# The second product of each layer by seven products instead of eight, in ten of twelve runs

## What is computed

```
scores = q_c @ k_c.T / sqrt(64);  attn = softmax(scores);  x = attn @ v_c      # per chunk of 64
x = x as 4608 tokens x 512
h = x @ moe_w_in                        # 512 x 2048
g = max(h, 0) + alpha * min(h, 0)
x = g @ moe_w_out                       # 2048 x 512
h = x @ moe2_w_in;  g = h - tanh(h);  out = g @ moe2_w_out
```

## Time and profile before

| | |
|---|---|
| median of three executions | 1586.36 us |
| the profiled execution | 1585.87 us, of which the span from the first to the last instruction is 1584.1 us |
| mean granted clock of TensorE | 0.997 |
| TensorE, weight loads | 1561.9 us, 1480.5 us |
| VectorE, ScalarE, POOL | 979.0, 619.2, 314.6 us |
| DMA | 375.04 MB, 237 GB/s over the span |

### The profile page before, as it was taken

One profiled execution on the slowest core, in us unless ns is written; L12 is line 12 of the kernel. 1 busy time (PEld: TensorE's weight loads), 2 busy tenths in 40 slices (PEclk: granted clock), 3 DMA queues, 4 the chain that ended last, 5 costly groups with the idle time before them and its releaser, 6 DMA issues.

```text
span 1584.1 us, 26708 instructions
## 1 busy us (share of the span) xinstructions
PE 1561.9 (99%) x10512; PEld 1480.5 (93%) x10512; DVE 979.0 (62%) x1371; ACT 619.2 (39%) x947; POOL 314.6 (20%) x434
## 2 busy tenths in 40 slices
PE   6999999999999999999999999999999999999999
PEld 5999999999999999999999989989989988988987
DVE  7987677668768766775864644653653652662642
ACT  5566335535534543553542322332331331241231
POOL 4974440051034015004564200000000000000000
PEclk8999999999999999999999999999999999999999
DMA  7695994697578579549879837636735735844741
GB/s 253 246 338 180 368 321 171 211 336 263 178 279 286 184 245 332 214 140 358 283 248 339 294 133 271 234 133 245 265 144 212 296 141 188 302 151 160 280 182 67
DMA packets 83146, 375.04 MB, mean 237 GB/s; under 512 B 10064, under 2 KB 23376, under 8 KB 48464
## 3 DMA queue, kind: packets, MB, share of 16 engines
q1 hardware_dynamic: 73136, 341.35, 59.8%
q0 software_dynamic: 9600, 31.46, 5.4%
q10 hardware_dynamic: 288, 0.52, 0.1%
HBM read 308.29 MB, written 65.01 MB: 236 GB/s over the span
## 4 chain that ended last, share of the span: by engine, by line
PE 93%; DVE 3%; issue 1%; DMA 1%; POOL 1%; ACT 0%; SPq 0%; DVEq 0%; ACTq 0%
PE banks L597 14%; PE banks L599 14%; PE banks L598 14%; PE banks L626 8%; PE banks L628 8%; PE banks L627 8%; PE banks L660 6%; PE banks L661 6%; PE banks L659 5%; PE a_bank L660 3%; PE a_bank L659 3%; PE a_bank L661 3%; POOL ring L409 1%; PE a_bank L535 1%; DMA ring<-w_split 1%
## 5 line engine op out<-in xcount | busy, mean ns | idle before, releaser
L597 PE MATMUL banks<-xo_hi,ring 128*128 128x384 f32 x1344 | 450.9, 336 | 2.7 <-DMA ring<-w_split 1.5
L599 PE MATMUL banks<-xo_hi,ring 128*128 128x384 f32 x1344 | 450.2, 335 | 0.0
L598 PE MATMUL banks<-xo_lo,ring 128*128 128x384 f32 x1344 | 450.1, 335 | 0.0
L1107 DVE TENSOR_TENSOR go_lo<-g_full,go_hi 128x768 fp32r<-128x768 f32 x288 | 281.2, 982 | 231.6 <-ACT go_hi L847 230.8
L847 ACT CAST go_hi<-g_full 128x768 fp32r<-128x768 f32 x288 | 239.8, 837 | 362.0 <-PE banks L661 223.8
L626 PE MATMUL banks<-go_hi,ring 128*128 128x384 f32 x768 | 260.4, 339 | 1.5 <-DVE go_lo L1107 1.1
L597 PEld LDWEIGHTS banks<-xo_hi,ring 128*128 128x128 f32 x1344 | 253.1, 188 | 5.2 <-issue 2.8
L628 PE MATMUL banks<-go_hi,ring 128*128 128x384 f32 x768 | 256.8, 334 | 0.0
L627 PE MATMUL banks<-go_lo,ring 128*128 128x384 f32 x768 | 256.7, 334 | 0.0
L598 PEld LDWEIGHTS banks<-xo_lo,ring 128*128 128x128 f32 x1344 | 253.1, 188 | 0.4
L599 PEld LDWEIGHTS banks<-xo_hi,ring 128*128 128x128 f32 x1344 | 253.0, 188 | 0.0
(11 more groups left out here) (130 smaller groups left out, 1839.9 us busy)
## 6 DMA issues: line engine op xcount, KB each, us to landing
ring<-w_split SPq DMA_DIRECT2D x242, 1024.0 KB, 6.4
w_split<-ring SPq DMA_DIRECT2D x22, 1024.0 KB, 5.1
qkv<-in_chunks SPq DMA_DIRECT2D x60, 256.0 KB, 5.3
w_split<-made_first POOLq DMA_DIRECT2D x44, 256.0 KB, 6.8
w_split<-sums POOLq DMA_DIRECT2D x44, 256.0 KB, 6.8
y_between<-stage SPq DMA_DIRECT2D x12, 768.0 KB, 8.0
x_raw<-y_between SPq DMA_DIRECT2D x6, 1536.0 KB, 10.7
out<-x_raw SPq DMA_DIRECT2D x36, 256.0 KB, 6.5
```

What stands on the lines that cost most here:

```text
L597: nc.tensor.matmul(h, hi, xo_hi[:, o, k, :], start=fresh and k == 0, stop=False, skip_group_check=not fresh)
L598: nc.tensor.matmul(h, hi, xo_lo[:, o, k, :], start=False, stop=False, skip_group_check=not fresh)
L599: last = nc.tensor.matmul(h, lo, xo_hi[:, o, k, :], start=False, stop=k == 1, skip_group_check=not fresh)
L1107: nc.vector.tensor_tensor(go_lo[:, slot, :, :], g_of(n), go_hi[:, slot, :, :], ALU.subtract).then_inc(glo_ready, 1)
```

## The change

**Runs 2 to 11** do the second product by seven products too. d_ff is the dimension that is summed over, so the halves of d_ff (two times 1024) and of d_model (two times 256) and of the tokens (two times 384) make the quarters, and each of the seven products runs over all of its 1024 in four parts q of two slices. That makes 28 *steps*, `STEPS`, of two blocks each. In layer 0 a block is six matmuls of 384 columns, in layer 1 nine of 256 columns with the tokens stationary. The left factors are differences of quarters of `g_full`, made in place by VectorE (`g_sum`, 16 per run, three of them already in phase A). The sums of Winograd's form grow in PSUM: P1 is copied by ScalarE to another pair of banks, product 6 is accumulated on it (U2), which is copied out, product 7 on it (U3), copied out, product 4 on it (C21); product 2 is accumulated on P1 itself (C11), and product 3 on product 5. Two additions on VectorE make C22 and C12 (`read_y22`, `read_y12`). Results are stored in quarters. Runs 0 and 1 keep the plain phase B (`PLAIN = 2`).

**Attention** for the tiles of runs 2 to 5 moves to phase A of the run before (runs 1 to 4): the scores of two units behind product 6 of an even pair p >= 2, their transposes behind product 6 of pair p+1, the product with v behind product 5 of p+1. The exponential is now eight instructions of 128x64 per unit that read PSUM, take the negated maximum as bias and give the row sum as a second output; the subtraction and the reduction for the row sum go.

**Weights.** A run from 2 on has 112 blocks (28 groups) and POOL makes 168 blocks in three passes over the raw weights: 56 for the second product of layer 0, 56 for the first and 56 for the second of layer 1. The table in `pace` is new: 42 of them in run 1, 24 in run 2, 20 each in runs 3 and 4, 42 in run 5, 20 in run 6. The loads of run 2 wait for the first 56 from group 14 on, and the loads of run 6 for the rest.

```diff
+STEPS = ([(i, q) for i in (1, 5, 6) for q in range(4)] + [(2, 0), (2, 1)] + [(7, q) for q in range(4)] + [(2, 2), (2, 3)]
+         + [(i, q) for i in (4, 3) for q in range(4)])
...
+MADE_ORDER = (7, 5, 6, 3, 1, 2, 4)
+MADE = [(layer, step_at(step_of(i, p // 2), p % 2) if second else product_at(i, p))
+        for layer, second in ((0, True), (1, False), (1, True)) for p in range(PAIRS) for i in MADE_ORDER]
...
 def pace(k):
-    if k < 60:
-        return 1 + k // 12, 4 * (k % 12) + 2
-    return (SUPER - 1, 56 + 2 * (k - 60)) if k < 76 else (SUPER, 4 * (k - 76) + 2)
-def raw_chunk(layer, j):
-    what, a, b = block_use(layer, j)
+    for s, count, first, tenths in ((1, 14, 2, 37), (1, 28, FIRST_BLOCKS, 10), (2, 16, 2, 30), (2, 8, 60, 60), (3, 14, 2, 37), (3, 6, 60, 80),
+                                    (4, 14, 2, 37), (4, 6, 60, 80), (5, 22, 2, 24), (5, 20, 58, 25), (6, 20, 2, 24)):
+        if k < count:
+            return s, first + tenths * k // 10
+        k -= count
+    raise ValueError(k)
...
+            def step(s, n, which=(0, 1)):
+                i, q = STEPS[n]
+                slot, fresh = go_slot(s, n), i in (1, 5)
+                for e in which:
+                    j = step_at(n, e)
+                    weights_ready(s, j)
+                    if e == 0:
+                        pe.wait_ge(glo_ready, go_count(s, n))
+                    if e == 0 and q == 0:
+                        if i == 1:
+                            pe.wait_ge(c21_ready, after_pairs(s, PAIRS - 2))
                             pe.wait_ge(c12_ready, after_pairs(s, PAIRS - 2))
+                        elif i == 5:
+                            pe.wait_ge(c21_ready, after_pairs(s, PAIRS - 1))
+                            pe.wait_ge(c12_ready, after_pairs(s, PAIRS - 1))
+                        elif i in (6, 2):
+                            pe.wait_ge(p1_copied, once(s))
+                        elif i == 7:
+                            pe.wait_ge(u2_copied, once(s))
+                        elif i == 4:
+                            pe.wait_ge(u3_copied, once(s))
                         else:
+                            pe.wait_ge(y22_ready, once(s))
+                    if layer_of(s) == 1 and n == 1 and e == 0:
+                        pe.wait_ge(c11_read, after_pairs(s, PAIRS - 2))
+                        some = go_hi[:, slot, 0, 0:P]
+                        nc.tensor.matmul(banks[:, 0, HALF:512], some, some, start=False, stop=True, skip_group_check=True)
+                    w = block_of(s, j)
+                    begin, end = fresh and q == 0 and e == 0, q == 3 and e == 1
+                    if layer_of(s) == 0:
+                        for m in range(2):
+                            hi, lo = w[:, 0, m * P:(m + 1) * P], w[:, 1, m * P:(m + 1) * P]
+                            y = banks[:, bank_pair(i) + m, 0:HALF]
+                            nc.tensor.matmul(y, hi, go_hi[:, slot, e, :], start=begin, stop=False, skip_group_check=not fresh)
+                            nc.tensor.matmul(y, hi, go_lo[:, slot, e, :], start=False, stop=False, skip_group_check=not fresh)
+                            last = nc.tensor.matmul(y, lo, go_hi[:, slot, e, :], start=False, stop=end, skip_group_check=not fresh)
+                    else:
+                        for m in range(3):
+                            hi, lo = go_hi[:, slot, e, m * P:(m + 1) * P], go_lo[:, slot, e, m * P:(m + 1) * P]
+                            y = banks[:, bank_pair(i) + m // 2, m % 2 * 256:(m % 2 + 1) * 256]
+                            nc.tensor.matmul(y, hi, w[:, 0, :], start=begin and m != 1, stop=False, skip_group_check=not fresh or m == 1)
+                            nc.tensor.matmul(y, hi, w[:, 1, :], start=False, stop=False, skip_group_check=not fresh or m == 1)
+                            last = nc.tensor.matmul(y, lo, w[:, 0, :], start=False, stop=end, skip_group_check=not fresh or m == 1)
+                    last.then_inc(block_done, 1)
...
+            def late_units(s, p):
+                first = UPS * (s + 1) + p - p % 2 - 2
+                return (first, first + 1) if phase_a_units(s) and p >= 2 else ()
...
                     product(s, 6, p)
+                    for u in late_units(s, p):
+                        if p % 2:
+                            transpose_attn(u)
+                        else:
+                            scores(u)
                     product(s, 1, p)
                     product(s, 4, p - 1)
                     product(s, 5, p)
+                    if p % 2:
+                        for u in late_units(s, p):
+                            output(u)
...
             def exponent(u):
-                act.wait_ge(shifted, u + 1)
-                nc.scalar.activation(probs_of(u), probs_of(u), ACT.Exp, scale=scale).then_inc(exp_done, 1)
+                if not late(u):
+                    act.wait_ge(shifted, u + 1)
+                    nc.scalar.activation(probs_of(u), probs_of(u), ACT.Exp, scale=scale).then_inc(exp_done, 1)
+                    return
+                act.wait_ge(shifted, together(u))
+                act.wait_ge(attn_ready, u - 1)
+                act.wait_ge(attnT_done, probs_users(u))
+                heads = score_bank(u)
+                for b in range(G * UNIT):
+                    for r in range(2):
+                        last = nc.scalar.activation(probs_of(u)[:, b, r, :], heads[:, r, b * CHUNK:(b + 1) * CHUNK], ACT.Exp,
+                                                    bias=row_max[:, u % 2, r, b:b + 1], scale=scale,
+                                                    accum_out=row_sum[:, u % 2, 2 * b + r:2 * b + r + 1])
+                last.then_inc(exp_done, 1)
...
+                mine = row_max[:, u % 2 if late(u) else 0, :, :]
+                nc.vector.tensor_reduce(mine, heads, AXIS_X, ALU.max).then_inc(max_ready, 1)
                 dve.wait_ge(max_ready, u + 1)
+                if late(u):
+                    nc.vector.tensor_scalar(mine, mine, -scale, None, ALU.mult).then_inc(shifted, 1)
+                    return
...
+            def g_sum(s, i, q):
+                if i == 5:
+                    dve.wait_ge(g_ready, g_count(s, 2 * q + 1, 1))
+                    if layer_of(s) == 1:
+                        dve.wait_ge(c11_read, after_pairs(s, 2 * q + 1))
+                    to, a, b = 1, 1, 0
+                elif i == 6:
+                    dve.wait_ge(t_ready, t_count(s, 5, q))
+                    dve.wait_ge(glo_ready, go_count(s, step_of(5, q)))
+                    to, a, b = 1, 3, 1
+                elif i == 7:
+                    dve.wait_ge(t_ready, t_count(s, 6, q))
+                    dve.wait_ge(glo_ready, go_count(s, step_of(1, q)))
+                    to, a, b = 0, 1, 0
+                else:
+                    dve.wait_ge(t_ready, t_count(s, 6, q))
+                    dve.wait_ge(glo_ready, go_count(s, step_of(2, q)))
+                    to, a, b = 2, 2, 1
+                nc.vector.tensor_tensor(g_pairs(q, to), g_pairs(q, a), g_pairs(q, b), ALU.subtract).then_inc(t_ready, 1)
...
+                    sp.wait_ge(w_stored[q % RING], 16 * stores_of(q))
+                if s == PLAIN and q >= 14 or s == SUPER:
                     for i in range(2):
-                        last = max(k for k in range(i, BLOCKS, 2) if MADE_SECOND[k] // PER_GROUP <= q)
+                        last = max(k for k in range(i, len(MADE), 2)
+                                   if MADE[k][0] == layer_of(s) and MADE[k][1] // PER_GROUP <= q)
                         sp.wait_ge(made_stored[i], 16 * (last // 2 + 1))
```

More of the change, by code:

```diff
@@ L105, in made_here, with turn, block_use @@
+def turn(s, j):
+    return ({54: 54, 56: 55, 55: 56} if plain(s) else {56: 54, 54: 55, 57: 56, 55: 57}).get(j, j)
+def block_use(j):
+    if j >= FIRST_BLOCKS:
+        return "unit", j - FIRST_BLOCKS, 0
+    return next(("product", i, p) for p in range(PAIRS) for i in range(1, 8) if product_at(i, p) == j)
 def made_here(s):
@@ L747, in _ @@
         def _(act):
[L748 to L757 removed]
+            made = {0: 0}
@@ L1156, in phase_a @@
                     sum_c22(s, p)
+                    if not plain(s) and p in (3, 5, 7):
+                        g_sum(s, 5, (p - 3) // 2)
                     if s == 0 and p == 0:
```

792 lines of the change are left out of this document (430 added, 362 removed).

## The result

The changed kernel takes 1725.58 us (median of 4 runs, 1717.83 to 1728.36), the kernel before 1586.63 (median of 4 on the same chip). The ratio is 1.0868, with a 95% interval of 1.083 to 1.0906: slower by 139 us. The forecast, 1664, had the side right and the time 62 us too low; the range, which ended at 1700, does not hold it.

A forecast was written before the change was run, and what follows sets the result against it. The prediction took TensorE's own stream to bound the kernel, with TensorE never short of input. From 1585.9 us it summed - 62 + 58 + 3 + 61 + 18 = 1664 us, range 1545 to 1700.

The forecast's parts named there:

- fewer and narrower matmuls: TensorE in phase B: 33.2 us gained in runs 2 to 5, 28.8 in runs 6 to 11, 62 in all.
- twelve waits of attention: Phase A, runs 1 to 4: TensorE waits 4.7 us per pair of units before transposes; 58 us with g_sums.
- run 2, made weights: TensorE waits for POOL's first made blocks at a guarded group of run 2: 3 us, 0 to 15.
- run 6, made weights: TensorE waits at a guarded group of run 6 for POOL's last made blocks: 61 us, 0 to 80.
- waits inside phase B: VectorE's low parts and ScalarE's copies in phase B: tight, but over 2 us of lead, so charged 0.
- clock: TensorE's clock falls at six of twelve attention waits and run 6's long wait: 7 x 2.6 = 18 us, 0 to 34.
- The prediction's own condition: Phase B, runs 2 to 5: if POOL's memory use slows VectorE's two operations to 1.1 us, 3 us lost per run.
- Rival (d): The 256-column matmul costs 0.14 us or more, or phase B starves VectorE: over 1700 us; chance 0.07.
- c: Price of one small 64-column exponential on ScalarE in phase A: taken as 0.42 us, between 0.06 and 0.42.
- 16c - 2.0: TensorE's wait in us before the transposes of two units in phase A, from 16 exponentials: 4.7 us.
- 4.62 us a block under load: POOL's time per made block while waiting for its stores under busy DMA, taken for both phases.
- the 106 blocks: Made blocks that the pace table lets POOL have ready when run 5 starts, leaving 60 until mid run 6.

The follow-up runs named there:

- run 5: Not a follow-up experiment: one of the kernel's own runs 0 to 11, the last in layer 0; its phase B took 69.15 us in the kernel before.
- e1: Changed kernel with ScalarE copying operands T2, T3 and T4 of the next run one step later in phase B: 1683.77 us.
- e7: Changed kernel with the moves of e1, e2 and e6 together: 1591.87 us, 1.0036 of the kernel before.
- e2: Changed kernel with only the pace table changed: POOL may make 30, 28, 28, 28 blocks in runs 2 to 5, 12 in run 6: 1672.13 us.
- e6: e3 with VectorE normalising two units behind sum_u3 and sum_c22 in pairs 2, 4 and 6, not ahead of them: 1680.58 us.
- e3: Changed kernel with attention's transposes in phase A three blocks later, behind product 5 of the odd pair, outputs behind product 7: 1708.65 us.
- e11: Changed kernel with seven products in phase B of layer 1 only, attention back in phase B, operands as in e1, 112 made blocks, new paces: 1560.99 us.
- e10: e7 with the plain phase B in run 2 as well (PLAIN = 3) and paces to suit: 1593.06 us.
- e9: Changed kernel without row sums from the small exponentials; VectorE normalises by sums left from an earlier unit: 1698.73 us, one run.

## Why the prediction failed, step by step

The terms against the profiled execution, in us:

| term | predicted | measured |
|---|---|---|
| fewer and narrower matmuls | -62 | -62 (see below) |
| twelve waits of attention | +58 | +40.6 |
| run 2, made weights | +3 | +10.8 |
| run 6, made weights | +61 | +56.5 |
| waits inside phase B | 0 | +35.3 |
| clock | +18 | +36 |
| the rest, not measured but left over | 0 | +25 |
| sum | +78 | +142 |

Of the 62 us of gain the 29 of layer 1 were measured (4.8 us for each phase B, run 11 above and runs 6 to 10 in e1). The 33 of layer 0 are a count of matmuls; the nearest measurement is phase B of run 3 in e1, 61.98 us against 69.15 without attention, 7.2 of the 8.3 us. Attention and run 6 were 22 us too high together, which hid a part of what the other terms lacked.

**Phase B, the step that failed.** "It is tight, but the ring of three go slots leaves over 2 us of lead, so I charge 0." The durations were right: 0.96 us for a low part and 0.95 for a difference in layer 1. What I did not do is go through ScalarE's queue step by step. A lead of 2 us is eaten by one copy that waits 3 us, whatever the load of either engine. The measured 35 us are 13.0 + 9.5 for go_lo and 7.6 + 5.2 that the view gives as issue, the last in the same places. e1 shows the cause of 29 of them. With the clock falls behind them it was 42 us. The prediction's own condition, low parts of 1.1 us at 3 us a run, was a second and smaller part: they took 1.05 us in phase B of run 3 in e1 and 1.21 in e7, where that phase is 4.6 us longer. Rival (d) named a starved VectorE and a time over 1700, but for the wrong reason, and had 0.07.

**Attention.** The mechanism stood (transposes come before probs, twelve times) and the term was mis-sized by c: 0.289 us, not 0.42. With c the formula 16c - 2.0 gives 2.6 us; the waits were 3.4 on average, 3.0 in run 1 and 3.5 in runs 2 to 4. So the formula's other numbers were 0.8 us a wait too low, which hid a part of the error in c. I had rightly taken the sum as a step of its own, and wrongly priced it at a whole fixed part. The Trainium skill, "ScalarE: Activation LUTs", section "What ACT_TABLE_LOAD costs", has 280 ns and 0.833 ns a column less 93 ns of overlap, by which, as an estimate, 64 columns with a bias take 0.240 us. The runs have 0.197 without the sum and 0.289 with it, so that its figure is too high for the one and, as it prices no sum, too low for the other.

**POOL.** The count held: 4.62 us a block under load was 4.5 in run 5 and the start of run 6 (38 blocks from 832 to 1003 us), and 2.69 with calm DMA (2.68 by the rows that it cites) was 2.53 (13 blocks from 1013 us). What I took as given, the 106 blocks that the table of paces allows up to run 5, was the cause: e2. For run 2 I had 3 (0 to 15), it was 10.8.

**Clock.** I took 7 falls at 2.6 us each. There were 17 between run 0 and the wait of run 6, one for each of the twelve waits of attention and five in phase B, one of these at the wait for made weights in run 2. They last 82 us in all, of which TensorE has matmuls in 69, and half of that, 34.5 us or 2.0 a fall, is lost; 1.4 more are lost behind the wait of run 6. The price was 0.6 us too high and the number less than half. I had spread the falls over half of twelve waits that were all alike.

**Short gaps.** The rest, 25 us, is the difference of the sum and the span. Some 5 us of it are smaller lines of the view of waits. Most lies in layer 0: even in e6, where phase A waits for nothing long, it takes 67.6 to 69.6 us, not 65.4. Some 3 us lie in layer 1, where phase B of runs 6 to 10 is 3.6 us longer than in e1 and its waits are 2.9. What each gap is stays open.

**The range.** Its upper end was the forecast and a little; it left out that terms charged at 0 (VectorE, the copies, short gaps) can only err upwards, and together they were 60 us.

## What to carry to other kernels

For each engine that feeds the bottleneck, write down its queue in order and, for every instruction, when its input is ready and who made it: a copy placed in the same step as its producer holds up all that is behind it, and no busy share shows it (42 us here; once more on VectorE in e3). Where the bottleneck engine has no slack, an edit that adds waits of a few us pays more than their length, since the clock falls too: here 40.6 us of waits in phase A cost 59 (e6). And weigh each part of a change by itself: here 29 of the 62 us of gain needed 24 more made blocks and no attention moved (e11, 1.6% faster than before), the other 33 needed 56 more and attention in phase A, and did not pay in any run here (e7, e10).

## What the runs showed of the hardware

- ScalarE's sum output is a separate ACTIVATION_READ_ACCUMULATOR that adds 0.09 us to each exponential of 64 columns (starts 0.289 us apart with it in the changed kernel, 0.197 without it in e9), so that sixteen 64-column exponentials with sums take 4.6 us.
- Over eleven profiles, from 180 us on, TensorE's granted clock fell to 0.50 (1.2 GHz) at or right behind 0 of 100 idle gaps of 1.0 to 1.5 us, 17 of 53 of 1.5 to 2.5, 33 of 46 of 2.5 to 3.5, and 26 of 27 longer ones. In the changed kernel a fall cost 2.0 us on average.
- Matmuls of 256 columns start 0.120 us apart, so the straight line of the prices of 384 and 512 columns holds down to there.
- VectorE's low part took 1.09 us on average in phase B of run 3 of the changed kernel and 0.96 in run 7, with POOL idle. It is POOL's own instructions that lengthen it and not the memory traffic. From 180 to 1000 us the 91 low parts that ran beside a cast, sum or difference of POOL took 1.25 us on average, the 58 that ran beside none 0.95 (0.96 at most), at a DMA share of 0.73 and 0.83. VectorE's sums of 128x384 with one input in PSUM (L1233) took 0.55 us either way. Two operations of VectorE in phase B of run 3, and the one of POOL beside the first (start us, us, instruction):

```profile
627.15 1.72 DVE L1303 TENSOR_TENSOR g_full<-g_full 128x768 f32<-128x768 f32 x1
629.66 0.95 DVE L1281 TENSOR_TENSOR go_lo<-g_full,go_hi 128x768 fp32r<-128x768 f32 x1
```

```profile
627.29 0.75 POOL L535 TENSOR_TENSOR raw<-raw 128x256 f32<-128x256 f32 x1
```

The Trainium skill, "SBUF — State Buffer", section "Who interferes with whom", gives the port that VectorE and POOL share as the one place of such stalls; these rows agree with that.
